# Windowed attention on one core: two triangular key spans merged into one square of scores per head, split again after one transpose

## What is computed

```python
batch, n_heads, seq, head_dim = (2, 8, 768, 64)
n_sink, window = (4, 128)

scores = scale * np.matmul(q, k.transpose(0, 1, 3, 2))
pos = np.arange(S)
is_sink = pos[None, :] < int(n_sink)
rel = pos[:, None] - pos[None, :]
in_window = (rel >= 0) & (rel < int(window))
keep = is_sink | in_window
scores = np.where(keep, scores, -1000000000.0)
scores = scores - np.max(scores, axis=-1, keepdims=True)
a = np.exp(scores)
a = a / (np.sum(a, axis=-1, keepdims=True) + 1e-09)
return np.matmul(a, v).astype(np.float32)
```

## Time and profile before

| | |
|---|---|
| median of 3 runs | 667.56 us |
| the runs | 663.25, 667.56, 669.09 us |
| profiled execution: span, first to last instruction | 658.6 us |
| profiled execution: time around the span | not in the profile |
| PE, DVE, ACT, POOL busy | 637.9, 328.8, 280.0, 185.5 us |
| granted TensorE clock, mean | 1.000 |
| attention | about 0 to 129 us of the span |

### The profile page before, as it was taken

How to read it: one execution, slowest core, us unless ns; L and a number is a source line. 1 busy time by engine, 2 the same in 40 slices (tenths; PEclk the granted TensorE clock), 3 DMA queues, 4 the chain that set the end, 5 groups by cost and what they waited for, 6 DMA issues and landing times.

```text
span 658.6 us, 11248 instructions
## 1 busy us (share of the span) xinstructions
PE 637.9 (97%) x3890; PEld 580.8 (88%) x3891; DVE 328.8 (50%) x691; ACT 280.0 (43%) x538; POOL 185.5 (28%) x199
## 2 busy tenths in 40 slices
PE   7999999898999999999999999999998999999997
PEld 6989999898999999999999999998777788888886
DVE  4466745587564726437164462556776612452211
ACT  5767866542353425244242433233633522442220
POOL 2501100125444351614516151300452121122111
PEclk9999999999999999999999999999999999999999
DMA  7867822173575564635646350350737911001000
GB/s 214 286 233 236 301 86 81 66 257 72 181 191 165 158 190 148 156 101 128 189 144 178 103 113 2 49 191 2 268 70 267 339 60 37 32 21 49 33 32 27
DMA packets 51090, 89.85 MB, mean 136 GB/s; under 512 B 7919, under 2 KB 14063, under 8 KB 51040
## 3 DMA queue, kind: packets, MB, share of 16 engines
q1 hardware_dynamic: 41872, 69.21, 30.8%
q0 software_dynamic: 9168, 19.97, 13.5%
HBM read 73.13 MB, written 17.02 MB: 137 GB/s over the span
## 4 chain that ended last, share of the span: by engine, by line
PE 87%; DMA 4%; DVE 3%; issue 2%; ACT 2%; SPq 1%; POOL 0%; another core or an unknown queue 0%; DVEq 0%; POOLq 0%; ACTq 0%
PE banks L1007 7%; PE banks L1006 7%; PE banks L1009 7%; PE banks L1067 6%; PE banks L1068 6%; PE banks L1086 6%; PE banks L811 5%; PE banks L839 5%; PE banks L1388 3%; PE banks L1358 3%; PE banks L1353 3%; PE banks L1384 3%; PE banks L1385 3%; PE banks L1354 3%; PE banks L823 2%
## 5 line engine op out<-in xcount | busy, mean ns | idle before, releaser
L1867 DVE TENSOR_TENSOR split<-stage,split 128x2048 fp32r<-128x2048 f32 x32 | 73.3, 2290 | 41.2 <-ACT split L1492 41.1
L1006 PE MATMUL banks<-xTs,split 128*128 128x416 f32 (+1 forms) x256 | 88.6, 350 | 0.4 <-issue 0.4
L1007 PE MATMUL banks<-xTs,split 128*128 128x416 f32 (+1 forms) x256 | 86.4, 342 | 0.0
L655 POOL DMA_INDIRECT x_moe<-rows,dst_idx x25 | 49.3, 1971 | 112.8 <-DVE rows L2320 111.9
L1067 PE MATMUL banks<-hTs,split 128*128 128x416 f32 x224 | 79.9, 357 | 0.0
L1068 PE MATMUL banks<-hTs,split 128*128 128x416 f32 x224 | 78.5, 350 | 0.0
L1627 ACT ACTIVATE hTs<-banks 128x416 fp32r<-128x416 f32 x56 | 29.0, 518 | 81.5 <-PE banks L1009 81.5
L1492 ACT ACTIVATE split<-stage 128x2048 fp32r<-128x2048 f32 x32 | 61.0, 1908 | 0.7 <-DMA stage<-w1a 0.7
L1009 PE MATMUL banks<-xTs,split 128*128 128x416 f32 (+1 forms) x256 | 56.2, 340 | 0.0
L1877 DVE CUSTOM_DVE_ANT_0 negs<-banks,masks 128x260 f32<-128x260 f32 (+2 forms) x96 | 35.0, 402 | 35.8 <-PE banks L811 34.6
L811 PE MATMUL banks<-k_sb,q_sb 128*128 128x260 f32 (+2 forms) x192 | 49.6, 384 | 3.3 <-DMA k_sb<-k_w 1.9
(11 more groups left out here) (378 smaller groups left out, 1285.0 us busy)
## 6 DMA issues: line engine op xcount, KB each, us to landing
stage<-w1a SPq DMA_DIRECT2D x16, 1024.0 KB
stage<-w2a SPq DMA_DIRECT2D x16, 1024.0 KB
k_sb<-k_w SPq DMA_DIRECT2D x12, 520.0 KB, 4.4
raw<-w1b SPq DMA_DIRECT2D x4, 1024.0 KB
raw<-w2b SPq DMA_DIRECT2D x4, 1024.0 KB
q_sb<-q_t SPq DMA_DIRECT2D x24, 128.0 KB, 3.5
x_attention<-rows SPq DMA_DIRECT2D x12, 256.0 KB, 5.8
split<-x_moe SPq DMA_DIRECT2D x12, 256.0 KB, 3.5
```

Source lines behind the costliest of these rows:

```text
L655: pool.indirect_dma_start(out=x_dram[1], out_offset=rows_at(dst_idx[0], early_dst, e, k), in_=y_lines(e, k), in_offset=None, compute_op=AL ...
L1006: pe.matmul(psum, piece(slot, 0, o + c * FH), xTs[:, 0, c, 0:cols], start=(c == 0), stop=False)
L1007: pe.matmul(psum, piece(slot, 1, o + c * FH), xTs[:, 0, c, 0:cols], start=False, stop=False)
L1867: dve.tensor_tensor(split_chunk(e % 2, 1, c), staged_chunk(e % 2, c), split_chunk(e % 2, 0, c).bitcast(F32), ALU.subtract).then_inc(low_do ...
```

## The change

It touches kind 2, blocks 2 to 5. PE writes the same 260 columns of scores. A predicated copy on DVE then writes, over the own block's scores, those of the block before wherever c > p (the constant `before`, which holds 1 there, read as 16-bit integers). What follows takes 132 columns, the square and the sinks: the mask is zero everywhere (`no_mask`), the exponentials are 132 wide, and one transpose for each head turns the square. In place of ACT's copy, DVE multiplies the turned square, out of PSUM, by each of two triangles of ones, which gives the two operands of the values in `pT`. The copy is linked. `split_sides` stands behind the masks in DVE's list and ahead of `sink_lows` and `normalize`. Two semaphores are merged into one (`set_ready`), and POOL prepares the new constants at the start.

```diff
@@ allocations
-            masks = sb_early("masks", [P, 3, WIN])
+            masks = sb_early("masks", [P, 2, WIN])
+            no_mask = sb_early("no_mask", [P, PACKED])
+            side_masks = sb_early("side_masks", [P, 2, P])
@@ gpsimd
-            select(masks[:, 2, 0:P], -1, -1, [[1, P]], MASKED, masks_ready)
-            select(masks[:, 2, P:2 * P], 0, 1, [[-1, P]], MASKED, masks_ready)
+            pool.memset(no_mask[:], 0.0).then_inc(masks_ready, 1)
+            pool.memset(side_masks[:], 1.0).then_inc(masks_ready, 1)
+            pool.wait_ge(masks_ready, 6)
+            select(side_masks[:, 0], -1, 1, [[-1, P]], 0.0, masks_ready)
+            select(side_masks[:, 1], 0, -1, [[1, P]], 0.0, masks_ready)
...
-                                 spread(probs[:, b, :, 2 * P:WIN], 1, COPIES)).then_inc(sink_packed, 1)
+                                 spread(probs[:, b, :, P:PACKED], 1, COPIES)).then_inc(sink_packed, 1)
@@ PE, transposes
                 pe.wait_ge(probs_ready, g * 2 + 2)
-                if kind > 0 or j >= 2:
+                if g >= 18:
+                    pe.wait_ge(sides, 2 * (g - 18) + 2)
+                elif kind > 0 or j >= 2:
                     pe.wait_ge(pt_copied, g - 1)
-                nb = 1 if kind == 0 else 2
+                nb = 2 if kind == 1 else 1
@@ PE, values
-                pe.wait_ge(pt_copied, g + 1)
+                if kind < 2:
+                    pe.wait_ge(pt_copied, g + 1)
+                else:
+                    pe.wait_ge(sides, 2 * (g - 16) + 2)
@@ ACT
+            def kept(kind):
+                return PACKED if kind == 2 else span(kind)
...
-                    act.activation(probs[:, b, 2 * pair + h, 0:span(kind)], negs[:, j % 2, h, 0:span(kind)], ACT.Exp,
+                    act.activation(probs[:, b, 2 * pair + h, 0:kept(kind)], negs[:, j % 2, h, 0:kept(kind)], ACT.Exp,
...
             def pt_copy(i, j, kind):
                 g = i * 8 + j
+                if kind == 2:
+                    return
@@ DVE, mask_scores
+                if kind == 2:
+                    link(dve.copy_predicated(S[:, j % 2, :, P:2 * P], spread(before[:].bitcast(U16), 1, 2), S[:, j % 2, :, 0:P]))
                 for h in range(2):
+                    if kind == 2:
+                        dve.tensor_tensor_reduce(out=negs[:, j % 2, h, 0:PACKED], in0=S[:, j % 2, h, P:WIN], in1=no_mask[:],
+                                                 scale=-SCALE, scalar=HUGE, op0=ALU.add, op1=ALU.min,
+                                                 accum_out=negmax[:, j % 2, h:h + 1]).then_inc(masked, 1)
+                        continue
@@ DVE, new
+            def split_sides(i, j):
+
+                g = i * 8 + j
+                dve.wait_ge(pt_ready, g + 1)
+                dve.wait_ge(pv_done, g - 1)
+                sides_of = pT[:, j % 2, :].rearrange("p (h k n) -> p k h n", h=2, k=2)
+                for k in range(2):
+                    dve.tensor_tensor(sides_of[:, k], PT[:, j % 2, 0:2 * P].rearrange("p (h n) -> p h n", h=2),
+                                      spread(side_masks[:, k], 1, 2), ALU.mult).then_inc(sides, 1)
@@ DVE, block_steps
                         mask_scores(i + 1, j - 6, next_kind)
+                    if kind == 2:
+                        split_sides(i, j)
                     prev = (i, 0) if b else (i - 1, 1)
```

More of the change, by code:

```diff
@@ L9 @@
 I32 = mybir.dt.int32
+U16 = mybir.dt.uint16
 ALU = mybir.AluOpType
@@ L21 @@
 WIN = 2 * P + SINK
+PACKED = P + SINK
 PAIRS = HEADS // 2
@@ L295, in build @@
         zero_ready = sem("zero_ready"); zeroed = sem("zeroed")
-        small_in = sem("small_in"); wg_in = sem("wg_in"); noise_in = sem("noise_in"); noise_ready = sem("noise_ready"); q_zeroed = sem("q_zeroed")
-        v_early = [sem(f"v_early{b}") for b in range(BATCH)]; ones_ready = sem("ones_ready"); v_late = sem("v_late"); vs_in = sem("vs_in"); vs_masked = sem("vs_masked"); vs_parted = sem("vs_parted")
+        small_in = sem("small_in"); wg_in = sem("wg_in"); noise_in = sem("noise_in"); noise_ready = sem("noise_ready");
+        v_early = [sem(f"v_early{b}") for b in range(BATCH)]; set_ready = sem("set_ready"); v_late = sem("v_late"); vs_in = sem("vs_in"); vs_masked = sem("vs_masked"); vs_parted = sem("vs_parted")
         qk_in = [sem(f"qk_in{b}") for b in range(BATCH)]
@@ L302, in build @@
         pt_ready = sem("pt_ready"); pt_copied = sem("pt_copied"); pv_done = sem("pv_done")
+        sides = sem("sides")
         sink_packed = sem("sink_packed"); sink_t = sem("sink_t"); sink_copied = sem("sink_copied"); sink_low = sem("sink_low")
@@ L939, in block_steps @@
                         x_logits(pi, pb)
-            pe.wait_ge(ones_ready, 1)
+            pe.wait_ge(set_ready, 1)
             keep_clock_up(REST_START)
-            pe.wait_ge(q_zeroed, 2)
+            pe.wait_ge(set_ready, 3)
             scores(0, 0, 0)
@@ L2002, in block_steps @@
                         sink_values_low(2 * j - 11)
-            dve.memset(ones_bf[:], 1.0).then_inc(ones_ready, 1)
+            dve.memset(ones_bf[:], 1.0).then_inc(set_ready, 1)
             for h in range(2):
-                dve.memset(q_sb[(1 - h) * HD:(2 - h) * HD, :, :, h, :], 0.0).then_inc(q_zeroed, 1)
-            dve.wait_ge(masks_ready, 6)
+                dve.memset(q_sb[(1 - h) * HD:(2 - h) * HD, :, :, h, :], 0.0).then_inc(set_ready, 1)
+            dve.wait_ge(masks_ready, 8)
             mask_scores(0, 0, 0)
```

## The result

| | before | after |
|---|---|---|
| median of 20 runs each, us | 666.82 (661.01 to 671.92) | 671.44 (666.19 to 678.71) |
| profiled execution, span, us | 658.6 | 675.5; a second one of the same kernel 663.5 |
| mean granted clock of TensorE in it | 1.00 | 0.983; 0.991 |
| sink values of block 5 on PE, us from the start | 128.48 | 137.25; 133.95 |

The change makes the kernel slower by a ratio of 1.0087, interval 1.0056 to 1.0118, some 3.7 to 7.9 us. Forecast were 671.4 us and, as the likeliest case, "within 1%": both came, though the upper end of the interval lies beyond 1%.

A forecast was written before the change was run, and what follows sets the result against it. PE was taken to bound a unit, with a 0.13 us DVE margin at sinkT. Blocks 2 to 4 +0.5 and block 5 +3.3 gave +3.8: span 662.4, plus 8.96, 671.4 us; range 666 to 677 (8 in 10).

The forecast's parts named there:

- within 1%: Whole kernel: measured time within 1% (6.7 us) of 667.6 us, chance 0.73.
- DVE's step and its place: Blocks 2 to 5: DVE takes 1.61 us per pair instead of 0.70; plain unit's sink values 2.11 us after pair 2's scores.
- The hand-over term: DVE's step: the mask waits for the linked copy's completion, 0.08 us, half of a 0.16 us idle row.
- the copy reads its target: Rival, every merged pair: copy costs 0.69 us, 0.27 more per step, together 9.5 us, 677.1 us; chance 0.17.
- No overlap: Rival, DVE's step: neighbouring instructions take full durations, 0.3 us more per step, about +10 us, 677.5 us; chance 0.06.
- Plain unit: Block 4: sink values 0.83 us late, PE idle 1.05, other pairs' transposes give back 0.66; net +0.17 us per unit.
- Units with low halves: Blocks 2 and 3, staged weights' low half on DVE (2.21 us): DVE is full, +0.2 us per unit.
- First unit of block 2: Block 2's start: pair 0's eviction, for which PE waited, goes; normalization delays values; PE 0.45 us ahead.
- Block 5: Block with the early choice of experts on DVE: 19.9 us to PE's restart against 16.67, +3.3 us.
- Sum: Attention: +0.5 us for blocks 2 to 4 plus 3.3 for block 5, +3.8 us, passed on whole.
- 8.96 around the span: Whole kernel: median 667.56 us lies 8.96 above the profiled span; added to the forecast span of 662.4 us.
- DVE stays hidden: Rival, all 32 pairs: copy and products finish within PE's other work, -7.0 us, 660.5 us; chance 0.07.

The follow-up runs named there:

- sinks first: Changed kernel with DVE subtracting sinkT's low half first in its step, ahead of the copy: median 669.43 us, ratio 1.0061 (1.0015 to 1.0108).
- the last version: Changed kernel, block 5 in two spans, DVE reordered (sinkT first, masks last), staged copy before exponentials, last zero rows stored behind block 4's loads: 655.96 us, 0.9926.
- changed, again: Second profiled execution of the changed kernel, nothing altered: span 663.5 us, one run of 666.59 us against 660.14.
- products between copy and masks: Changed kernel with DVE running a pair's two products between the copy and the masks: median 668.29 us, ratio 1.0102 (1.0049 to 1.0154).

## Why the prediction was right, and where it was not

*DVE's step and its place.* Right: 1.57 us against 1.61, and from the end of pair 2's scores to the sink values 2.05 (100.61 to 102.66) against 2.11; PE waits 1.01 against 1.05. The hand-over term (0.08, bounded by 0.16) was 0.03. That the copy's target is not read at a price of its own is shown by its 427 ns; "the copy reads its target" (690) fell. "No overlap" fell too: masks of 293 ns start 220 apart. The prediction took only half of what the Trainium skill ("VectorE: DVE Perf Modes", section on the DRAIN) says: the next instruction waits for an empty pipe, but one that is not held starts earlier. These rows agree with the second half. The same page's section on the TRN2 errata gave an estimated 390 ns for the copy, by its row for PSUM to SBUF; the measured 427 decides.

*Plain unit.* +0.28 against +0.17. The rest of the unit, from the sink values to the end of pair 2's scores, took 8.83 instead of 8.66: the sink values take 0.50 there against 0.42 in the chain before, the values after them 0.91 against 0.84.

*Units with low halves.* The failed step: "They meet: DVE is full, and the unit is +0.2 us". It is +0.53. They do meet: pair 2's products end at 73.84, and PE, without a wait, would ask for them at 73.90. But PE's wait of 0.27 at the transpose of the sinks (L863) was missing: I followed only what DVE owes PE for pair 2 and sinkT, not the small copy of the logits queued behind these products (73.76). And "DVE is full" was wrong: "sinks first" brings these units to 10.28.

*Last unit of block 4.* +0.51 against +0.17: two memsets (L2054, L2055) and the first instruction of the early choice (L1960) stand between the products and DVE's next copy there, 108.52 to 109.26 us, and PE waits 1.25 for sinkT instead of 1.01. Not counted at all.

*First unit of block 2.* Forecast -0.45. Its first sink values come 0.83 later than before, where -0.45 and the 0.83 for sinkT implied 0.38. From the scores in block 2's first step to them it takes 13.64 us (42.25 to 55.89) against 13.36 (41.70 to 55.06), +0.28 and so near the forecast; the value products wait 0.66 for the normalized rows, behind masks and products on DVE. The other 0.55 is there when these scores start, and it is not the merge: with blocks 2 and 3 in two spans they start at 42.76, and in the kernel before slowed in block 5 alone, the same code up to there, at 42.52.

*Block 5.* 14.27 against 14.30, tail 8.40 against 8.33 + 0.13. Restored alone, it returned 3.46 us of attention.

*Sum.* Attention +5.5 instead of +3.8, with the excess up to the end of block 4, 0.55 of it there before block 2's first step. That it passes on whole is likely but not shown: 529.6 against 530.1 us behind it is a net of half clock and a shorter wait, and the first execution took 538.3. Measured are +4.6 between the medians, 5.8 by the ratio. "8.96 around the span" was a wrong reading: times lie 1.7 to 3.2 us above spans in every run, and the profiled execution of before, with a clock of 1.00, was a quick one. In 671.4 a shift too small by 0.8 us meets a median before taken 0.7 us too high (667.56, with 20 runs 666.82). That the forecast came to 0.04 us is luck; its size is better than its working.

*"DVE stays hidden"* fell with the first wait for sinkT; it would have needed the order of the last version, and there units are 9.8 to 10.0 us, where that rival has 10.60 - 0.88 = 9.72. The triangle products are no loss in themselves: their place in DVE's queue, ahead of what PE wants next, was.

*Open.* In the first, second and fourth batch kernels with a merged block 5 were granted a lower mean clock (0.983 to 0.991) than before or those with an old block 5 (0.994 to 0.996). Of eight profiles with a merged block 5, seven show a drop of 3.4 to 17.1 us in or just behind block 5 (all but "sinks first"), of six others none, beside drops at other places that most profiles have. In the third batch the mean clock was 0.9895 to 0.992 for all four kernels, and it is 0.988 for the 20 runs after; for the 20 before it was not recorded. Idle time of the same length did not bring the drop to the kernel before, and filling it did not take it from the changed one. So the stretches show what DVE's queue costs in attention, but some of the measured 5.8 us may be clock; how much, and what sets it off, these runs do not settle.

## What to carry to other kernels

Work moved to an engine at half load is not free when it lands in a queue ahead of the one small result that the bounding engine asks for next: lay out that engine's queue by the order in which its results are wanted (here sinkT, copy, products, normalization, masks last), and after each repair look for the next late one (normalized rows, then ACT's staged copy, then a load behind stores). A share of busy time below one does not show that there is room. And read gaps off a timeline: a piece of a chain may lie inside an instruction.

## What was not expected of the hardware

- A predicated copy of 128x256 within PSUM, with a two-byte mask, takes 427 ns, as a plain two-operand product of that size does (418).
- A semaphore hand-over from DVE to DVE costs 0.03 us; what it loses is the overlap of neighbours, 0.12 (copy to mask 0.46, copy to product 0.34).
- TensorE fell to 1.2 GHz for 3.4, 6.8 or 17.1 us at a time. In "changed, again" it had last waited 0.97 us, until 117.99, before the drop at 119.4; with its waits filled (20.48 busy of 21.00 us) it fell all the same, at 134.0. In the 17.1 us of "products between copy and masks" it stayed at 1.2 GHz though busy for 15.9 of them.
- The same kernel before had medians of 660.14 to 660.46 us in three batches and 667.32 in the other, on another chip.
